# A second buffer for transposed probabilities, an earlier copy, and a layer norm with interleaved subtractions: a transformer sequence block on one Trainium2 core

## The chip, the cores and the metric

The kernel runs on one core of one Trainium2 chip. The metric is device time in microseconds (us), the median of several runs. The five engines are TensorE (PE; its weight loads are shown as PEld), VectorE (DVE), ScalarE (ACT), GpSimd (POOL) and SyncE (SP, which here only issues DMAs). Each engine takes its instructions in the order in which the kernel gives them, and they wait for each other with semaphores.

## The reference

```python
scores = (q @ k.T) / sqrt(D), masked        # 4 batches, 8 heads, 576 tokens, D = 64
attn = exp(scores - rowmax); attn /= attn.sum()
x = heads side by side of (attn @ v)        # [4, 576, 512]
h = gelu(x @ w_in); u, v = halves of h      # 512 each
v_n = (v - mean) / sqrt(var + 1e-6) * g_ln  # layer norm over 512 features
v_s = w_sg @ v_n + b_sg                     # "spatial": mixes the 576 tokens
x = x + (u * v_s) @ w_out
xn = layer norm of x * g2
out = x + relu(xn @ w_ch1) @ w_ch2          # 2048 hidden features
```

Heads 0 to 3 see a local window of 32 tokens, heads 4 to 7 see earlier tokens of the same class (position modulo 32).

## The kernel before

Every product but those of attention is done in three matmuls: each operand is split in a rounded part (hi) and the rest (lo), and hi*hi, hi*lo and lo*hi are summed in PSUM (lines 935 to 937). Making a lo part is one subtraction on DVE or POOL.

Attention of one batch is cut in 24 blocks of 90 to 108 queries for two heads; two blocks make a twin, so a batch has 12 twins, 3 for each pair of heads. A twin s goes through these steps: `scores` (PE, 4 matmuls, line 959), `maxima` (DVE, masked scores to SBUF and row maxima, 722), `exps` (ACT, 4 exponentials and their row sums, 528), `normalise` (DVE, reciprocal 730 and 4 scalings 735), `transposes` (PE, into the one bank `pT_bank`, 972), `copy_pT` (ACT, from that bank to the SBUF tile `probsT`, 538), `values` (PE, into `pv_bank`, 986), `copy_x` (545 on ACT for even twins, 742 on DVE for odd ones) and, once for each pair, `round_x` (DVE, 749) and `split_x` (POOL, 385), which give the operands xop_hi and xop_lo of the next product.

The attention of batch 0 has nothing to run beside it: this is the solo stage, with 15 steps (`SOLO_STEPS`). In step s PE does scores of twin s, transposes of twin s-2 and values of twin s-3, with some warm-up matmuls on zeros (line 943) in steps 0 to 7. A part of the v projection is put between transposes and values in steps 8, 9, 11, 12 and 14 (`SOLO_V`): a v part (k, tokens) is three matmuls, for pair k and one tile of 128 tokens, and needs xop_lo of pair k. The list `REST_V` holds the v parts that SOLO_V does not name; they follow the solo stage. The five v groups (tiles of tokens) are then complete, eight u groups follow, and their Gelu runs on ACT.

Then comes the layer norm of v in five tiles (`norm_all_v` on DVE: `v_stats` lines 753 and 756, `v_norm` lines 760 and 763; on POOL `root_v`, lines 392 and 395, and `split_v`, line 400). In POOL's queue before it stand split_x and the four `split_win` of the u half (line 374); in DVE's queue before it stand four casts (710) and `split_wsg`, the five subtractions that split the spatial weights w_sg (830 and 835). The first mix group (the product with w_sg) waits for all five wsg_lo and for all five vn_lo. On PE the scores of twin 0 of the next batch stand just ahead of it.

From there on, the attention of batch b+1 is interleaved with the mix and out groups of batch b (`period`), by the lists `AFTER_T` and `AFTER_P`: each step holds scores, transposes, one or two groups, and values. DVE finishes a mix group in `gate` (770 and 774), POOL makes gated_lo (407). In the first period POOL also splits w_out (379) right after the layer norm. After four batches comes the feed-forward product in six tiles of 384 tokens, the larger part of the span.

Of the kernel before, what the change touches and what calls it, by code (L numbers as in the profile page):

```python
# [16 lines left out]
F32 = mybir.dt.float32  # L17
F32R = mybir.dt.float32r
BF16 = mybir.dt.bfloat16
ALU = mybir.AluOpType  # L20
# [3 lines left out]
P = 128  # L24
# [29 lines left out]
for _pair in range(PAIRS // 2, PAIRS):  # L54
    for _i, _n in enumerate(CLASSES):
# [5 lines left out]
TWINS = NT // 2  # L61
# [4 lines left out]
NS = -(-S // P)  # L66
LAST = S - (NS - 1) * P
# [18 lines left out]
LAG = 2  # L86
STEPS = TWINS + LAG
# [1 line left out]
SOLO_LAG = LAG + 1  # L89
SOLO_STEPS = TWINS + SOLO_LAG  # L90

SOLO_V = {8: ((0, 0), (0, 1)), 9: ((0, 2), (0, 3)), 11: ((1, 0), (1, 1)), 12: ((1, 2), (1, 3)),
          14: ((2, 0), (2, 1))}

def warm_steps(s):
    return 3 if s < LAG else 2 if s < min(SOLO_V) else 0


REST_V = [(k, s) for k in range(KC) for s in range(NS - 1) if (k, s) not in sum(SOLO_V.values(), ())]
AFTER_T = [(0,), (1,), (2,), (3,), (5,), (6,), (7,), (8,), (10,), (11,), (12,), (13,), (14,), (15,)]  # L100
# [5 lines left out]
def sequence_block_kernel(nc, qT, kT, vW, w_in, g1, w_sgT, b_sg, w_out, g2, w_ff, masks, eye, out):  # L106
    with ExitStack() as ctx:
        def sb(name, shape, dt=F32, stack=ctx):
            return stack.enter_context(nc.sbuf_tensor(name, shape, dt))

        def sem(name):
            return ctx.enter_context(nc.semaphore(name))
# [8 lines left out]
        phase_a = ExitStack()  # L121
# [1 line left out]
        k_sb = sb("k_sb", [P, PAIRS, KPAD], F32, phase_a)  # L123
        v_sb = sb("v_sb", [P, NT, P], F32, phase_a)
        probs = sb("probs", [P, 3, 4 * P], F32, phase_a)
        probsT = sb("probsT", [P, 4 * P], F32, phase_a)
        win_hi = sb("win_hi", [P, KC, 2 * GATE], F32R, phase_a)
        win_lo = sb("win_lo", [P, KC, 2 * GATE], F32R, phase_a)
        xop_hi = sb("xop_hi", [P, KC, S], F32R, phase_a)
# [3 lines left out]
        wsg_hi = sb("wsg_hi", [P, NS, S], F32R, phase_a)  # L133
# [34 lines left out]
        wsg_raw_last = res[:, S:2 * S]  # L168
# [37 lines left out]
        mask_in, class_mask_in, eye_in, const_in = sem("mask_in"), sem("class_mask_in"), sem("eye_in"), sem("const_in")  # L206
# [7 lines left out]
        win_hi_ready, wrest_hi_ready = sem("win_hi_ready"), sem("wrest_hi_ready")  # L214
        wa_lo = sem("wa_lo")
        wsg_lo_ready = sem("wsg_lo_ready")
# [6 lines left out]
        pv_ready = sem("pv_ready")  # L223
# [51 lines left out]
        pT_bank, pv_bank = bank[2], bank[3]  # L275
# [26 lines left out]
        def settle(engine):  # L302
            engine.sem_inc(waited, 1)
# [219 lines left out]
        def _(act):  # L523
            def exps(b, s):
                for j in range(2):
                    act.wait_ge(max_ready, b * NT + (2 * s + j + 1))
                    for h in range(2):
                        last = act.activation(probs_at(s, j, h), probs_at(s, j, h), ACT.Exp, scale=-1.0,  # L528
                                              bias=stat_at(neg_max, s, j, h),
                                              accum_out=stat_at(row_sum, s, j, h))  # L530
                    last.then_inc(exp_done, 1)

            def copy_pT(b, s):
                _, nq, nk, _, _, _ = BLOCKS[2 * s]
                if s >= 1:
                    act.wait_ge(pv_ready, b * TWINS + s)
                act.wait_ge(pT_ready, b * TWINS + (s + 1))
                act.activation(probsT[0:nk, 0:4 * nq], pT_bank[0:nk, 0:4 * nq],
                               ACT.Copy).then_inc(pT_copied, 1)

            def copy_x(b, s):
                dst, src = heads_out(b, s)
                act.wait_ge(pv_ready, b * TWINS + (s + 1))
                settle(act)
                act.activation(dst, src, ACT.Copy).then_inc(x_even, 1)
# [102 lines left out]
                norm_hi(0, 0)  # L648

            for s in range(SOLO_STEPS):  # L650
                if s < TWINS:
                    exps(0, s)
                if LAG <= s < STEPS:
                    copy_pT(0, s - LAG)
                if s >= SOLO_LAG and s % 2 == SOLO_LAG % 2:
                    copy_x(0, s - SOLO_LAG)
            period(0, first=True)
# [37 lines left out]
        def _(dve):  # L695
# [16 lines left out]
            def maxima(b, s):  # L712

                _, nq, nk, _, _, _ = BLOCKS[2 * s]
                dve.wait_ge(scores_ready, b * TWINS + (s + 1))
                if s >= 3:
                    dve.wait_ge(pT_ready, b * TWINS + (s - 2))
                settle(dve)
                for j in range(2):
                    mask = mask_b[0:nq, BLOCKS[2 * s + j][5], 0:nk]  # L720
                    for h in range(2):
                        last = dve.tensor_tensor_reduce(out=probs_at(s, j, h), in0=scores_at(s, j, h),  # L722
                                                        in1=mask, scale=-SCALE, scalar=3.0e38, op0=ALU.add,
                                                        op1=ALU.min, accum_out=stat_at(neg_max, s, j, h))
                    last.then_inc(max_ready, 1)
# [25 lines left out]
            def v_stats(b, s):  # L751
                dve.wait_ge(gelu_done, b * NGELU + (s + 1))
                dve.bn_stats(bn6[:, s, :], gv[:, s, :]).then_inc(bn_done, 1)
                dve.wait_ge(bn_done, b * NS + (s + 1))
                settle(dve)
                dve.bn_aggr(mean_var[:, s, :], bn6[:, s, :]).then_inc(aggr_done, 1)

            def v_norm(b, s):
                dve.wait_ge(rstd_done, b * NS + (s + 1))
                dve.tensor_scalar(gv[:, s, :], gv[:, s, :], mean_var[:, s, 0:1],  # L760
                                  rstd_v[:, s:s + 1], ALU.subtract, ALU.mult).then_inc(vn_done, 1)
                dve.wait_ge(vn_done, b * NS + (s + 1))
                dve.tensor_copy(vn_hi[:, s, :], gv[:, s, :]).then_inc(vnh_ready, 1)
# [20 lines left out]
            def empty_group(b, i):  # L784
                if i < NMIX:
                    gate(b, i)
                else:
                    add_out(b, i - NMIX)
# [28 lines left out]
                    dve.tensor_tensor(w_lo[f][:, part], w_raw[:, f % 2, part], w_hi[f][:, part].bitcast(F32),  # L817
                                      ALU.subtract).then_inc(done, 1)

            def norm_all_v(b):  # L820
                for s in range(NS + 1):
                    if s < NS:
                        v_stats(b, s)
                    if s >= 1:
                        v_norm(b, s - 1)

            def split_wsg():
                for s in range(NS - 1):
                    dve.wait_ge(wrest_hi_ready, s + 1)
                    dve.tensor_tensor(wsg_lo[:, s, :], wsg_raw[:, s, :],  # L830
                                      wsg_hi[:, s, :].bitcast(F32), ALU.subtract).then_inc(wsg_lo_ready, 1)

                dve.wait_ge(wrest_hi_ready, NS)
                second = wsg_hi[LAST:P, NS - 1, :]
                dve.tensor_tensor(second, wsg_raw_last[LAST:P, :], second.bitcast(F32),
                                  ALU.subtract).then_inc(wsg_lo_ready, 1)
                dve.wait_ge(const_in, 48)

            def period(b, first=False):
                if first:  # L840
                    split_wsg()
                norm_all_v(b)
                for s in range(STEPS):
                    if s < TWINS:
                        maxima(b + 1, s)
                    if 1 <= s <= TWINS:
                        normalise(b + 1, s - 1)
                    if s % PER_PAIR == LAG and s > LAG:
                        round_x(b + 1, s // PER_PAIR - 1)
                    for i in AFTER_T[s]:  # L850
                        empty_group(b, i)
                    if s >= LAG and s % 2 != LAG % 2:
                        copy_x(b + 1, s - LAG)
                    for i in AFTER_P[s]:
                        empty_group(b, i)
                round_x(b + 1, PAIRS - 1)
# [73 lines left out]
        def _(pe):  # L930
# [44 lines left out]
            def values(b, s):  # L975
                _, nq, nk, _, _, _ = BLOCKS[2 * s]
                if s % PER_PAIR == 0:
                    pe.wait_ge(v_in[s // PER_PAIR], (b + 1) * 16)
                if s >= 1:
                    wait_copied(pe, b, s - 1)  # L980
                pe.wait_ge(pT_copied, b * TWINS + (s + 1))
                settle(pe)
                for j in range(2):
                    for h in range(2):
                        rows = slice(h * D, (h + 1) * D)
                        last = pe.matmul(pv_bank[rows, j * nq:(j + 1) * nq], v_sb[0:nk, 2 * s + j, rows],  # L986
                                         probsT[0:nk, (2 * j + h) * nq:(2 * j + h + 1) * nq], start=True, stop=True)
                last.then_inc(pv_ready, 1)

            def v_part(b, s, chunks, first=False):  # L990
# [111 lines left out]
            for s in range(SOLO_STEPS):  # L1102
# [7 lines left out]
                warm_up(warm_steps(s) - warm_steps(s) // 2)  # L1110
                for k, tokens in SOLO_V.get(s, ()):
                    v_part(0, tokens, (k,), first=True)
# [122 lines left out]
```

## Time and profile before

| | |
|---|---|
| time, median of 3 runs | 736.11 us (732.35 to 737.01) |
| the profiled execution, time | 732.36 us |
| the profiled execution, span | 730.6 us |
| PE busy | 712.1 us (97%) |
| DVE, ACT, POOL busy | 331.6, 251.5, 195.8 us |
| mean granted clock of TensorE | 0.997 of full |

The span runs from the first to the last instruction that the profile shows; the time has 1.8 us more around it. Times in rows are microseconds from the span's start. Busy PE time is modelled, since matmuls overlap.

### The profile page before, as it was taken

The page shows a single profiled execution, that of the slowest core. Times are in us where ns is not written, and L with a number is a line of the kernel's source. Part 1 is how long each engine was busy: PE and PEld are TensorE (multiplying, and loading weights), DVE is VectorE, ACT ScalarE, POOL GpSimd, SP SyncE. Part 2 cuts the span into 40 slices and gives each one's busy share as a digit, 9 for nine tenths or more (in the row PEclk, how much of TensorE's full clock was granted, in tenths as well). Part 3 has the DMA queues.
Part 4 walks back from the last instruction along what each step waited for, and adds up shares of the span by engine and source line. Part 5 has one row for each costly group of instructions (what it writes and reads, how often), then busy time and mean ns, then how long its engine had stood idle before and what let it go on. Part 6 is the DMA issues. An engine that isn't in the chain of part 4 may idle for free.

```text
span 730.6 us, 12914 instructions
## 1 busy us (share of the span) xinstructions
PE 712.1 (97%) x4768; PEld 669.4 (92%) x4768; DVE 331.6 (45%) x1032; ACT 251.5 (34%) x738; POOL 195.8 (27%) x194
## 2 busy tenths in 40 slices
PE   8778999999999999999999999999999999999998
PEld 4558888988898888999999999999999999999998
DVE  6857883688468846673442231223222222322112
ACT  6754563376337634434431211122112112121110
POOL 1347321622162236463350203020201302010000
PEclk9999999999999999999999999999999999999999
DMA  8541004200420010024301000100100010001001
GB/s 300 205 164 58 1 1 142 80 2 1 132 89 0 0 58 1 31 74 145 126 33 44 1 1 0 44 1 1 44 1 1 0 44 1 1 1 44 1 0 44
DMA packets 15992, 35.02 MB, mean 48 GB/s; under 512 B 1728, under 2 KB 5696, under 8 KB 15936
## 3 DMA queue, kind: packets, MB, share of 16 engines
q1 hardware_dynamic: 15936, 34.29, 13.3%
q8 instruction: 34, 0.56, 0.3%
q14 instruction: 22, 0.18, 0.1%
HBM read 29.56 MB, written 4.72 MB: 47 GB/s over the span
## 4 chain that ended last, share of the span: by engine, by line
PE 91%; DVE 4%; POOL 2%; issue 2%; ACT 1%; DVEq 0%; POOLq 0%; ACTq 0%
PE bank L935 27%; PE bank L937 27%; PE bank L936 27%; PE bank L959 3%; PE bank L986 3%; PE bank L972 3%; DVE probs L722 1%; DVE probs L735 1%; DVE wsg_lo L830 1%; PE bank L943 1%; PE bank L1049 1%; PE bank L1050 1%; POOL rstd_v L395 0%; POOL vn_lo L400 0%; ACT probs L528 0%
## 5 line engine op out<-in xcount | busy, mean ns | idle before, releaser
L898 DVE SCALAR_TENSOR_TENSOR hid_lo<-bank,hid_hi 128x384 fp32r<-128x384 f32 x96 | 53.5, 557 | 281.0 <-ACT hid_hi L664 281.0
L664 ACT ACTIVATE hid_hi<-bank 128x384 fp32r<-128x384 f32 x96 | 47.1, 491 | 300.7 <-PE bank L937 300.7
L936 PE MATMUL bank<-xn_lo,w_hi 128*128 128x384 f32 x384 | 129.5, 337 | 0.0
L937 PE MATMUL bank<-hid_hi,w_lo 128*128 128x384 f32 x384 | 129.5, 337 | 0.0
L935 PE MATMUL bank<-hid_hi,w_hi 128*128 128x384 f32 x384 | 129.4, 337 | 0.0
L937 PE MATMUL bank<-xn_hi,w_lo 128*128 128x384 f32 x384 | 129.2, 336 | 0.0
L935 PE MATMUL bank<-xn_hi,w_hi 128*128 128x384 f32 x384 | 129.0, 336 | 0.0
L936 PE MATMUL bank<-hid_lo,w_hi 128*128 128x384 f32 x384 | 128.9, 336 | 0.0
L528 ACT ACTIVATE probs<-probs,stat 96x128 f32<-96x128 f32 (+2 forms) x192 | 71.9, 377 | 9.6 <-DVE stat L722 9.4
L935 PEld LDWEIGHTS bank<-hid_hi,w_hi 128*128 128x128 f32 x384 | 72.2, 188 | 0.0
L937 PEld LDWEIGHTS bank<-xn_hi,w_lo 128*128 128x128 f32 x384 | 72.1, 188 | 0.0
L935 PEld LDWEIGHTS bank<-xn_hi,w_hi 128*128 128x128 f32 x384 | 72.1, 188 | 0.0
L936 PEld LDWEIGHTS bank<-hid_lo,w_hi 128*128 128x128 f32 x384 | 72.1, 188 | 0.0
L936 PEld LDWEIGHTS bank<-xn_lo,w_hi 128*128 128x128 f32 x384 | 72.1, 188 | 0.0
L937 PEld LDWEIGHTS bank<-hid_hi,w_lo 128*128 128x128 f32 x384 | 72.0, 188 | 0.0
L722 DVE CUSTOM_DVE_ANT_0 probs<-bank,mask_b 96x128 f32<-96x128 f32 (+2 forms) x192 | 41.1, 266 | 20.0 <-PE bank L959 18.9
L440 POOL TENSOR_TENSOR xn_lo<-xc,xn_hi 128x1536 fp32r<-128x1536 f32 x6 | 21.1, 3511 | 100.2 <-ACT xn_hi L597 100.2
L735 DVE TENSOR_SCALAR probs<-probs,stat 96x128 f32<-96x128 f32 (+2 forms) x192 | 46.1, 299 | 1.8
L407 POOL TENSOR_TENSOR gated_lo<-u_sb,gated_hi 128x288 fp32r<-128x288 f32 x32 | 27.2, 854 | 62.7 <-ACT gated_hi L574 62.7
L385 POOL TENSOR_TENSOR xop_lo<-res,xop_hi 128x576 fp32r<-128x576 f32 x16 | 22.7, 1416 | 78.1 <-DVE xop_hi L749 78.1
L935 PE MATMUL bank<-wsg_hi,vn_hi 128*128 128x288 f32 x128 | 40.3, 315 | 3.1 <-POOL vn_lo L400 3.1
L935 PE MATMUL bank<-gated_hi,wout_hi 128*128 128x288 f32 x128 | 39.9, 311 | 0.0
(97 smaller groups left out, 1338.7 us busy)
## 6 DMA issues: line engine op xcount, KB each, us to landing
w_raw<-w_ff_dram SPq DMA_DIRECT2D x16, 512.0 KB, 3.5
v_sb<-vW_dram SPq DMA_DIRECT2D x16, 384.0 KB, 6.7
k_sb<-kT_dram SPq DMA_DIRECT2D x15, 304.0 KB, 6.8
q_sb<-qT_dram SPq DMA_DIRECT2D x15, 288.0 KB, 6.5
out_dram<-res SPq DMA_DIRECT2D x5, 768.0 KB, 3.9
res<-w_sgT_dram SPq DMA_DIRECT2D x1, 1152.0 KB, 10.7
win_v_raw<-w_in_dram SPq DMA_DIRECT2D x4, 256.0 KB, 6.8
win_u_raw<-w_in_dram SPq DMA_DIRECT2D x4, 256.0 KB, 8.7
```

The source lines that it names most:

```text
L385: pool.tensor_tensor(xop_lo[:, pair, :], res_at(b, pair, 0, S), xop_hi[:, pair, :].bitcast(F32), ALU.subtract).then_inc(x_lo, 1)
L407: pool.tensor_tensor(gated_lo[:, c, cols], u_sb[:, c, cols], gated_hi[:, c, cols].bitcast(F32), ALU.subtract).then_inc(gl_ready, 1)
L528: last = act.activation(probs_at(s, j, h), probs_at(s, j, h), ACT.Exp, scale=-1.0, bias=stat_at(neg_max, s, j, h), accum_out=stat_at(row_s ...
L664: act.activation(hid_hi[:, f % 2, :], h_bank[f % 2][:, 0:TILE], ACT.Relu).then_inc(hh_ready, 1)
L722: last = dve.tensor_tensor_reduce(out=probs_at(s, j, h), in0=scores_at(s, j, h), in1=mask, scale=-SCALE, scalar=3.0e38, op0=ALU.add, op1=A ...
L735: last = dve.tensor_scalar(e, e, stat_at(row_inv, s, j, h), None, ALU.mult)
L898: dve.scalar_tensor_tensor(out=hid_lo[:, f % 2, :], in0=h_bank[f % 2][:, 0:TILE], scalar=0.0, in1=hid_hi[:, f % 2, :].bitcast(F32), op0=AL ...
L935: pe.matmul(dst, wh, xh, start=(start and i == 0), stop=False)
L936: pe.matmul(dst, wh, xl, start=False, stop=False)
L937: last = pe.matmul(dst, wl, xh, start=False, stop=(stop and i == n - 1))
L959: last = pe.matmul(scores_at(s, j, h), q_sb[rows, pair, q0:q0 + nq], k_sb[rows, pair, k0:k0 + nk], start=True, stop=True)
L972: last = pe.transpose(pT_bank[0:nk, cols], probs_at(s, j, h), eye_f[0:nq, 0:nq])
```

## The change

- `probsT` gets two buffers; twin s uses number s % 2. `copy_pT` of twin s then waits for the values of twin s-2 instead of s-1, in all periods.
- In the solo stage ACT does `copy_pT` of twin s-2 ahead of `exps` of twin s; it stood behind them. In the other periods the copy stood ahead already.
- The five subtractions for w_sg no longer precede the layer norm of v in DVE's queue. One follows each of its iterations. The wait for the constants moves behind the layer norm.
- The two v parts of step 14 of the solo stage go to `REST_V`, behind it.

```diff
-SOLO_V = {8: ((0, 0), (0, 1)), 9: ((0, 2), (0, 3)), 11: ((1, 0), (1, 1)), 12: ((1, 2), (1, 3)),
-          14: ((2, 0), (2, 1))}
+SOLO_V = {8: ((0, 0), (0, 1)), 9: ((0, 2), (0, 3)), 11: ((1, 0), (1, 1)), 12: ((1, 2), (1, 3))}
...
-        probsT = sb("probsT", [P, 4 * P], F32, phase_a)
+        probsT = sb("probsT", [P, 2, 4 * P], F32, phase_a)
...
             def copy_pT(b, s):
-                if s >= 1:
-                    act.wait_ge(pv_ready, b * TWINS + s)
+                if s >= 2:
+                    act.wait_ge(pv_ready, b * TWINS + (s - 1))
                 act.wait_ge(pT_ready, b * TWINS + (s + 1))
-                act.activation(probsT[0:nk, 0:4 * nq], pT_bank[0:nk, 0:4 * nq],
+                act.activation(probsT[0:nk, s % 2, 0:4 * nq], pT_bank[0:nk, 0:4 * nq],
...
             for s in range(SOLO_STEPS):
+                if LAG <= s < STEPS:
+                    copy_pT(0, s - LAG)
                 if s < TWINS:
                     exps(0, s)
-                if LAG <= s < STEPS:
-                    copy_pT(0, s - LAG)
...
-            def norm_all_v(b):
+            def norm_all_v(b, first=False):
                 for s in range(NS + 1):
                     if s < NS:
                         v_stats(b, s)
                     if s >= 1:
                         v_norm(b, s - 1)
+                    if first and s < NS:
+                        split_wsg(s)
...
             def period(b, first=False):
+                norm_all_v(b, first)
                 if first:
-                    split_wsg()
-                norm_all_v(b)
+                    dve.wait_ge(const_in, 48)
```

## Rows read from the trace of the kernel before

**Rows 1.** Waits of PE over the whole span: total us, times, longest us.

```profile
PE bank L972 <- ACT probsT L538: 5.1, 9, 1.0
...
PE bank L935 <- POOL xop_lo L385: 2.7, 2, 1.4
```

**Rows 2.** Windows: length, busy PE, PEld, DVE, ACT, POOL, PEclk, DMA share, GB/s.

```profile
71.30:74.50 3.20, 3.20 (x19) 2.64 (x17) 0.96 (x2) 0.00 (x0) 3.20 (x4) 0.50 0.02 5
...
200.00:260.00 60.00, 60.00 (x515) 53.38 (x513) 45.03 (x199) 35.30 (x132) 20.35 (x25) 1.00 0.09 33
```

**Rows 3.** Timeline of ACT, solo stage: start, us, instruction, idle before and its releaser.

```profile
11.40 0.47 ACT L538 ACTIVATE probsT<-bank 128x384 f32<-128x384 f32 x1
...
39.67 0.47 ACT L538 ACTIVATE probsT<-bank 90x360 f32<-90x360 f32 x1 [2.25 <-PE bank L986]
```

**Rows 4.** Timeline of PE, solo stage to the first mix groups.

```profile
12.01 0.52 PE L972 MATMUL bank<-eye_f,probs 96*128 96x96 f32 x4 [0.63 <-ACT probsT L538]
...
25.26 0.55 PE L972 MATMUL bank<-eye_f,probs 108*108 108x108 f32 x4 [1.54 <-DVE probs L735]
...
34.05 0.55 PE L972 MATMUL bank<-eye_f,probs 108*108 108x108 f32 x4 [1.01 <-ACT probsT L538]
...
37.19 0.48 PE L972 MATMUL bank<-eye_f,probs 90*90 90x90 f32 x4 [0.72 <-ACT probsT L538]
...
39.03 0.59 PE L986 MATMUL bank<-probsT,v_sb 108*64 108x108 f32 x8
...
42.68 0.47 PE L935 MATMUL bank<-win_hi,xop_hi 128*128 128x512 f32 x1 [1.34 <-POOL xop_lo L385]
...
44.24 0.53 PE L986 MATMUL bank<-probsT,v_sb 90*64 90x90 f32 x8
...
47.75 0.47 PE L935 MATMUL bank<-win_hi,xop_hi 128*128 128x512 f32 x1 [1.39 <-POOL xop_lo L385]
...
53.72 0.40 PE L935 MATMUL bank<-xop_hi,win_hi 128*128 128x288 f32 x1 [0.23 <-POOL win_lo L374]
...
70.45 0.37 PE L935 MATMUL bank<-wsg_hi,vn_hi 128*128 128x288 f32 x1 [3.13 <-POOL vn_lo L400]
```

**Rows 5.** Timeline of DVE, solo stage: the scalings of twins 1 and 9.

```profile
10.36 0.87 DVE L735 TENSOR_SCALAR probs<-probs,stat 96x128 f32<-96x128 f32 x4
...
32.46 0.83 DVE L735 TENSOR_SCALAR probs<-probs,stat 108x108 f32<-108x108 f32 x4
```

**Rows 6.** Timeline of DVE: three w_sg subtractions (narrow windows), then the layer norm's start.

```profile
50.67 1.85 DVE L830 TENSOR_TENSOR wsg_lo<-res,wsg_hi 128x576 fp32r<-128x576 f32 x1
...
54.20 1.42 DVE L830 TENSOR_TENSOR wsg_lo<-res,wsg_hi 128x576 fp32r<-128x576 f32 x2
...
56.44 0.69 DVE L753 BATCH_NORM_STATS2 bn<-gv 128x6 f32<-128x512 f32 x1
...
57.38 0.66 DVE L753 BATCH_NORM_STATS2 bn<-gv 128x6 f32<-128x512 f32 x1
...
58.58 0.55 DVE L760 TENSOR_SCALAR gv<-gv,mean_var,rstd_v 128x512 f32<-128x512 f32 x1 [0.20 <-POOL rstd_v L395]
59.16 0.43 DVE L763 CAST vn_hi<-gv 128x512 fp32r<-128x512 f32 x1
```

**Rows 7.** Timeline of POOL: u half of w_in, then vn_lo of tiles 1, 2 and 4.

```profile
47.57 6.10 POOL L374 TENSOR_TENSOR win_lo<-win_u_raw,win_hi 128x512 fp32r<-128x512 f32 x4
...
62.09 1.29 POOL L400 TENSOR_TENSOR vn_lo<-gv,vn_hi 128x512 fp32r<-128x512 f32 x1
...
64.53 1.28 POOL L400 TENSOR_TENSOR vn_lo<-gv,vn_hi 128x512 fp32r<-128x512 f32 x1
...
69.04 1.26 POOL L400 TENSOR_TENSOR vn_lo<-gv,vn_hi 128x512 fp32r<-128x512 f32 x1 [0.82 <-DVE vn_hi L763]
```

**Rows 8.** Timeline of DVE and PE: the first gate's product, the first period's first transposes.

```profile
74.05 1.51 DVE L774 TENSOR_TENSOR u_sb<-gt,u_sb 128x288 f32<-128x288 f32 x1
...
77.73 0.52 PE L972 MATMUL bank<-eye_f,probs 96*128 96x96 f32 x4 [0.42 <-DVE probs L735]
```

More of the change, by code:

```diff
@@ L825, in norm_all_v, with split_wsg @@
                         v_norm(b, s - 1)
-            def split_wsg():
-                for s in range(NS - 1):
-                    dve.wait_ge(wrest_hi_ready, s + 1)
+                    if first and s < NS:
+                        split_wsg(s)
+            def split_wsg(s):
+                dve.wait_ge(wrest_hi_ready, s + 1)
+                if s < NS - 1:
                     dve.tensor_tensor(wsg_lo[:, s, :], wsg_raw[:, s, :],
                                       wsg_hi[:, s, :].bitcast(F32), ALU.subtract).then_inc(wsg_lo_ready, 1)
[L833 to L837, printed above, removed]
+                else:
+                    second = wsg_hi[LAST:P, NS - 1, :]
+                    dve.tensor_tensor(second, wsg_raw_last[LAST:P, :], second.bitcast(F32),
+                                      ALU.subtract).then_inc(wsg_lo_ready, 1)
             def period(b, first=False):
+                norm_all_v(b, first)
                 if first:
-                    split_wsg()
-                norm_all_v(b)
+                    dve.wait_ge(const_in, 48)
                 for s in range(STEPS):
@@ L986, in values @@
                         last = pe.matmul(pv_bank[rows, j * nq:(j + 1) * nq], v_sb[0:nk, 2 * s + j, rows],
-                                         probsT[0:nk, (2 * j + h) * nq:(2 * j + h + 1) * nq], start=True, stop=True)
+                                         probsT[0:nk, s % 2, (2 * j + h) * nq:(2 * j + h + 1) * nq], start=True, stop=True)
                 last.then_inc(pv_ready, 1)
```

## The prediction

> **What bounds the kernel now.** I read the waits of PE first. PE is busy 712.1 of 730.6 us, so the change can only give back idle time, and nearly all of that is early: 5.1 us in nine waits of transposes for the copy of the transposed probabilities and 2.7 us in two waits of v parts for xop_lo [rows 1], and 3.13 us in one wait of the first mix group for vn_lo [rows 4]. The windows say where the reader should look: after 80 us PE shows no idle time until the last tail, one short wait aside (60.00 busy in the window of 60.00 between 200 and 260 us) [rows 2]. So every microsecond by which PE reaches the steady part earlier should come off the end, and the changed wait of `copy_pT` in the later periods is worth nothing, since there no PE instruction waits for it. The windows show one more loss: right after the wait of 3.13 us [rows 4] the granted clock is 0.50 (1.2 GHz) from 71.30 to 74.50 [rows 2]. Shorter PE waits, up to 1.54 us [rows 4], are followed by no such fall. At half clock those 3.20 us hold work of 1.6.
>
> The timelines then show the chains. In the solo stage the copy of twin 0 starts at 11.40, behind the exponentials of twin 2, and transposes 1 start at 12.01 after it [rows 3, 4], though their own data left DVE at 10.36 + 0.87 = 11.23 [rows 5]. At the end of the stage there are no exponentials any more, but each copy waits for the values before it (copy 10 after 2.25 us of idle time ended by line 986) [rows 3], each transposes for the copy, and each values for its place behind v parts: a ring of three engines.
>
> **The change part by part.** I walk along PE and note by how much each landmark of [rows 4] comes sooner (its shift).
>
> 1. Copy ahead of exponentials. Transposes 1 can start 0.11 after the scalings, at 11.34 instead of 12.01: shift 0.7. What is late next is DVE's own order (maxima, scalings), which sets the pace up to transposes 6: these wait 1.54 us for the scalings, not for a copy [rows 4], so the shift there is still 0.7 and the other early copy waits give nothing. The exponentials are now queued behind the copy (0.38 of ACT's time each step) and behind the transposes it waits for. I cost that at nothing, as the scalings of a twin come a whole step later on DVE, and at 0.4 for twins 2 and 8 at worst.
>
> 2. Two buffers. Transposes 7 and 8 lose short waits, 0.35 together (part of the nine): shift 1.05. Transposes 9 at 34.05 waited 1.01 for copy 8. Without that they wait for scalings 9, which end at 32.46 + 0.83 = 33.29 [rows 5], plus 0.11, less the 1.0 by which the twin is early: 32.4, shift 1.6. From 9 to 10 there is then only PE work: 3.14 apart less the 0.72 of waiting [rows 4] gives 2.42, so transposes 10 start at 34.8 and values 9 (1.84 behind them as before) at 36.6: shift 2.4. Transposes 11 follow at 37.1, copy 11 at 37.7 while values 10 run, values 11 at 38.3 instead of 44.24: shift 5.9. The 5.9 includes the 1.5 us of two v parts that no longer stand ahead of it.
>
> 3. The two v parts. They need xop_lo of pair 2, which hangs on values 9 through copy_x 9, round_x and split_x. They now start at 42.68 - 2.4 = 40.3. Four parts of pair 2 (0.70 each, from two in about 1.4) take PE to 43.1. xop_lo of pair 3 hangs on values 11 and comes at 47.75 - 5.9 = 41.8, under them. So the wait of 1.39 goes and pair 3's parts start at 43.1: shift 4.65. A wait of about 1.5 us stays between values 11 and 40.3. The u groups lose a further 0.23 of waiting for win_lo, if that is ready: it ended at 47.57 + 6.10 = 53.67 [rows 7], hangs on values 11 too, and so comes at 47.8, ahead of the u groups at 48.85 (shift 4.9). PE was ready for the first mix group at 70.45 - 3.13 = 67.32 [rows 4] and would be at 62.45.
>
> 4. Subtractions in the layer norm. Before, DVE did them from 50.67 to 56.4 and only then the statistics [rows 6]. Now statistics 0 start when Gelu of the first v group is done, near 44.8, and the gate is POOL: its win_lo ends at 47.8, rstd of tile 0 is there a microsecond later, near 48.8 (the same two POOL operations fill the 1.15 between the end of vn_lo 1 at 63.38 and vn_lo 2 [rows 7]). From there the chain is scalings and cast of tile 0 (1.1), a subtraction of 0.7 (two in 1.42 where nothing collides) [rows 6], vn_lo 0 to 51.65, then three turns, then 2.1 for the last tile: vn_lo 3 to vn_lo 4, as now. A turn took 64.53 - 62.09 = 2.44 [rows 7], set by POOL, with DVE waiting inside it. DVE's work in a turn (0.94 from one statistics to the next, 0.55 scalings, 0.43 cast, 0.71 subtraction [rows 6]) is 2.6, so I take 2.65. Three turns give 59.6, the last tile 61.7, the mix group 61.85: 0.6 ahead of PE. Bounds: 2.44 a turn if it hides fully (61.2), and 0.94 + 0.55 + 0.43 + 1.85 = 3.8 if each subtraction, tile 0's too, takes the 1.85 of the colliding one at 50.67 [rows 6] (a mix group at 51.65 + 1.15 + 3 x 3.8 + 2.1 + 0.15 = 66.4). I stay near the low end, because that row collided with POOL subtractions back to back, 6.10 us for four, and in the layer norm POOL runs one of 1.29 per turn [rows 7].
>
> The rows show what a collision is: two subtractions, one on DVE and one on POOL, never progress together; 1.85 is 1.2 of waiting and 0.7 of work. The Trainium skill ("SBUF — State Buffer", "Who interferes with whom") says the same as a rule: a DVE instruction with two SBUF inputs and a GpSimd instruction that reads SBUF take an exclusive lock, and the second one is fully blocked. It speaks against this edit, since it moves DVE's subtractions from beside win_lo to beside vn_lo. By that rule a turn is at least the locked work of both, which gives an estimate of about 2.9 to 3.0 and a mix group at 62.8, 0.4 late on PE; without any lock, 2.6 and no wait.
>
> 5. First period. With the mix group at 62.45 (shift 8.0) the 3.13 wait is gone and so, by the only case there is, the fall of the clock: 1.6 more. It isn't all kept. At full clock DVE is late: the first gate's product took 1.51 [rows 8], beside POOL's splits of w_out, which still follow vn_lo. Mix group 0 ends at 64.4, gate to 66.45, maxima 1 to 67.4, scalings 0 to 68.4, transposes 0 at 68.55 instead of 77.73 [rows 8]: shift 9.2. If the gate's product doesn't collide, 67.7 and a shift of 10.
>
> From transposes 0 on the steps are those of before. The sum: 2.4 (attention until values 9), 2.25 (v parts), 0.25 (win_lo), 3.1 (layer norm), 1.2 (clock, less DVE's lateness) = 9.2. I take 9.1. The profiled execution, 732.36 with a span of 730.6, would become 723.3. It is near the lowest of the runs; the median is 3.75 above it. I take the saving off the median: 736.1 - 9.1 = **727.0**.
>
> **The rivals.** (a) The layer norm stays last. With turns of 3.8 the mix group starts at 66.4, PE waits 4.0 us, the clock falls again, and the gain ends where it stands at that group: 4.0, time 732.1. For it: the 1.85 row and the one wide vector instruction more in every turn. Against: POOL is free of subtractions for half a turn. A turn of 3.1 costs only 0.7 and stays in my range.
>
> (b) The solo stage is held by DVE and ACT, not by copies. Before, transposes 6 wait for DVE [rows 4]; if scalings 9 to 11 come late too (exponentials behind copies, scalings that collide with POOL), values 11 gain 3 instead of 5.9, win_lo and the layer norm follow, and the gain is 5 to 6: time 730.5.
>
> (c) Slower. The clock falls ahead of the u groups. The two v parts no longer fill the wait for xop_lo at the end of the solo stage, and PE idles there. I get 1.5 us; the clock fell after 3.13 and not after 1.54 [rows 4], so it decides if round_x or split_x of pair 2 come 1.5 us later relative to values 11. If the clock then stayed at half for all of the v parts and u groups, 40.3 to 62.4, that would be 22 us more, and 749. For it: PE has idle time all through this stage. Against: the one fall of the trace lasted 3.2 us and cost 1.6, and that much would leave 728.6. Only a long fall makes it slower.
>
> (d) The second buffer doesn't act: there is still one `pT_bank`, so transposes s+1 wait for copy s anyway. That wait is now only the copy's 0.47 after the transposes, under other PE work except at twins 10 and 11, so I give the buffer its effect. If it fell out, parts 1, 3 and 4 remain, some 5 us: 731.
>
> **How the numbers follow.** Forecast, gain 7.4 to 10.5: 0.66. (a) 0.11. (b) and (d) together, 4 to 7.3: 0.17. (c) 0.03. No visible effect because something unseen takes its place: 0.03. The range reaches from the highest gain on the lowest level of the runs (732.4 - 10.5 = 722) to (a) and (b) on the median's level, 732. A measurement of this kernel tells about 1% (7.4 us) from no change. Faster by over 1%: 0.65; within 1%: 0.32, from (a), (b), (d) and the low end of the forecast; slower: 0.03.
>
> **What would show it.** Right: no PE wait for line 538 in twins 9 to 11 of the solo stage; values 11 near 38.3; one wait for xop_lo left, of about 1.5 us; the wait for vn_lo under 1 us; granted clock 1.00 around the first mix group; transposes 0 of the first period near 68.6; every later landmark earlier by the same amount. Wrong: subtractions of 1.8 us each inside the layer norm, with vn_lo turns over 3.5; a wait of transposes for line 735 that grows in twins 9 to 11; a half clock anywhere between 38 and 62 us.

## The result and the profile after

The changed kernel takes 724.43 us (median of 4 runs, 724.2 to 725.51) against 734.23 (4 runs, 732.28 to 737.01) for the kernel before. The ratio is 0.9867, with a 95% interval of 0.9825 to 0.9909. In a later set of runs on one chip it was 726.28 against 734.78, ratio 0.9886 (0.9862 to 0.9910). The profiled executions have spans of 722.4 and 730.6 us: 8.2 less, where the prediction said 9.1 to 9.2.

The waits of PE in the changed kernel, over the whole span (lines have moved up by one: 971 are transposes, 985 values, 958 scores, 934 to 936 the three products):

```profile
PE bank L971 <- issue: 2.8, 4, 1.6
PE bank L958 <- DVE stat L721: 1.9, 5, 0.5
...
PE bank L985 <- ACT res L544: 1.0, 2, 0.7
PE bank L985 <- DVE res L741: 0.7, 1, 0.7
PE bank L971 <- DVE probs L734: 0.5, 1, 0.5
```

Of the three kinds of wait of [rows 1] and [rows 4] none is left: no transposes wait for the copy, no v part for xop_lo, and the mix group doesn't wait for vn_lo. The transposes that wait with no releaser shown ("issue") are those of twins 1, 4, 6 and 9, the 1.6 being that of twin 6, which waited for DVE's scalings before [rows 4]. One kind has grown: scores wait for DVE's maxima, 1.9 us in five waits where it was 0.8 in two; this is the other ring of the solo stage. One is new: values wait for `copy_x`, lines 544 and 741. The prediction had one wait for xop_lo of about 1.5 us left. There is none, because values 11, 1.5 us later than it said, stand in that time.

The timelines of DVE (first line, the scalings of twin 9) and PE show where each landmark of [rows 4] went:

```profile
31.57 0.83 DVE L734 TENSOR_SCALAR probs<-probs,stat 108x108 f32<-108x108 f32 x4
...
32.50 0.55 PE L971 MATMUL bank<-eye_f,probs 108*108 108x108 f32 x4 [0.35 <-issue]
...
36.72 0.59 PE L985 MATMUL bank<-probsT,v_sb 108*64 108x108 f32 x8
...
38.49 0.53 PE L985 MATMUL bank<-probsT,v_sb 90*64 90x90 f32 x8 [0.74 <-DVE res L741]
39.77 0.53 PE L985 MATMUL bank<-probsT,v_sb 90*64 90x90 f32 x8 [0.75 <-ACT res L544]
40.37 0.50 PE L934 MATMUL bank<-win_hi,xop_hi 128*128 128x512 f32 x1
...
44.78 0.39 PE L934 MATMUL bank<-win_hi,xop_hi 128*128 128x512 f32 x1
...
50.28 0.29 PE L934 MATMUL bank<-xop_hi,win_hi 128*128 128x288 f32 x1
...
63.70 0.40 PE L934 MATMUL bank<-wsg_hi,vn_hi 128*128 128x288 f32 x1
...
69.56 0.52 PE L971 MATMUL bank<-eye_f,probs 96*128 96x96 f32 x4 [0.46 <-DVE probs L734]
```

| landmark | before | walked in the prediction | after |
|---|---|---|---|
| transposes 9 | 34.05 | 32.4 | 32.50 |
| values 9 | 39.03 | 36.6 | 36.72 |
| values 11 | 44.24 | 38.3 | 39.77 |
| first v part of pair 2 behind the stage | 42.68 | 40.3 | 40.37 |
| first v part of pair 3 | 47.75 | 43.1 | 44.78 |
| u groups | 53.72 | 48.85 | 50.28 |
| first mix group | 70.45 | 62.45 | 63.70 |
| transposes 0, first period | 77.73 | 68.55 | 69.56 |

The last row is 8.17 us earlier and the end 8.2: behind it nothing was gained or lost, as PE has no idle time there.

The clock did not stay at full. The window of the changed kernel that answers to that of [rows 2] (same columns) is

```profile
40.60:44.00 3.40, 3.40 (x9) 2.69 (x9) 3.27 (x5) 3.07 (x5) 2.29 (x2) 0.51 0.69 224
```

PE's clock was 0.51 of full here (the third number from the end). The fall behind the layer norm is gone and another stands here, after a stretch (37.2 to 40.4) of short PE work with waits of 0.74 and 0.75. A half clock anywhere between 38 and 62 us was one of the prediction's own signs of being wrong.

The layer norm of v with its subtractions, DVE (two turns) and POOL:

```profile
51.14 0.75 DVE L831 TENSOR_TENSOR wsg_lo<-res,wsg_hi 128x576 fp32r<-128x576 f32 x1
...
53.71 0.75 DVE L831 TENSOR_TENSOR wsg_lo<-res,wsg_hi 128x576 fp32r<-128x576 f32 x1
...
56.27 0.75 DVE L831 TENSOR_TENSOR wsg_lo<-res,wsg_hi 128x576 fp32r<-128x576 f32 x1
```

```profile
43.10 6.13 POOL L373 TENSOR_TENSOR win_lo<-win_u_raw,win_hi 128x512 fp32r<-128x512 f32 x4
...
51.30 1.74 POOL L399 TENSOR_TENSOR vn_lo<-gv,vn_hi 128x512 fp32r<-128x512 f32 x1
...
54.19 1.42 POOL L399 TENSOR_TENSOR vn_lo<-gv,vn_hi 128x512 fp32r<-128x512 f32 x1
...
61.70 1.29 POOL L399 TENSOR_TENSOR vn_lo<-gv,vn_hi 128x512 fp32r<-128x512 f32 x1 [0.83 <-DVE vn_hi L762]
```

A subtraction takes 0.75, not 1.85; vn_lo pays for it, 1.74 and 1.42 instead of 1.29. A turn is 2.57 (51.14 to 53.71, and again to 56.27). The last vn_lo ends at 61.70 + 1.29 = 62.99, 0.7 us ahead of the first mix group at 63.70.

Behind the mix group, DVE's first gate product and the scalings of twin 0:

```profile
66.41 0.62 DVE L773 TENSOR_TENSOR u_sb<-gt,u_sb 128x288 f32<-128x288 f32 x1
...
68.00 1.42 DVE L734 TENSOR_SCALAR probs<-probs,stat 96x128 f32<-96x128 f32 x4
```

### The profile page after: what moved, and what is told of

Read it like the earlier page. It is cut to its first block, busy times and chain, and to the rows that moved or that the text cites. A ratio compares the mean times of both kernels' runs of the same rounds, so it can differ in the third digit from the quotient of the medians.

```text
span 722.4 us, 12909 instructions
## 1 busy us (share of the span) xinstructions
PE 710.7 (98%) x4766; PEld 669.7 (93%) x4768; DVE 327.9 (45%) x1032; ACT 251.4 (35%) x738; POOL 197.0 (27%) x194
## 4 chain that ended last, share of the span: by engine, by line
PE 95%; DVE 3%; issue 1%; POOL 1%; ACT 0%; DVEq 0%; POOLq 0%; ACTq 0%
PE bank L934 28%; PE bank L935 28%; PE bank L936 28%; PE bank L958 3%; PE bank L985 3%; PE bank L971 3%; DVE probs L721 1%; DVE probs L734 1%; PE bank L1048 1%; PE bank L942 1%; PE bank L1049 1%; PE bank L1054 0%; DVE res L905 0%; PE bank L1055 0%; POOL acc L419 0%
```

## The experiments

Times vary by up to 3 or 4 us between executions of one kernel, and the first thing to learn from the runs was why. "Half clock" below is a granted clock of 0.50, which is 1.2 GHz. Each execution comes with its mean granted clock. Spans of the executions for which that clock is on record, by clock:

| kernel | 1.000 | 0.998, 0.997 | 0.995 | 0.993 | 0.991 |
|---|---|---|---|---|---|
| before | | 730.5 to 731.3 | 731.4 to 733.1 | 732.2 to 734.4 | 734.4 to 734.6 |
| changed | | 722.4 to 722.7 | 723.7 to 725.4 | | |
| v parts kept | | 725.7 to 726.1 | 727.7 | | |
| exponentials first | 723.7 | | 725.4 | 726.4, 726.9 | |
| one buffer | | | 727.2, 727.3 | 728.0, 728.1 | |
| w_sg first | | 725.2 | 725.8, 726.5 | 727.6 | |
| attention only | | 728.8 | 729.0 to 729.6 | 730.5 | |
| spread only | 726.7 | 727.7, 728.1 | 729.6 to 730.1 | | |
| v parts only | | | 729.4, 729.7 | 730.0 to 731.2 | 731.1 |
| other pv bank | 721.3 | 722.2 | 723.6 | 724.9 | |
| warm-up in the tail | 722.3, 722.7 | 723.5, 724.0 | | | |
| bank and warm-up | 721.3 to 721.6 | | 724.2, 724.3 | | |
| more warm-up | 721.4 to 721.6 | | | | |

The windows of the profiled executions show what a column means: 1.000 has no half clock, 0.998 one stretch of some 3.4 us, 0.995 twice as much in all (in two stretches, or in one of 6.8 us), 0.993 three times. Within a row, each 3.4 us at half clock go with 0.8 to 1.7 us more. So I compare within a column. That still leaves up to 2 us open, as in the row of the changed kernel at 0.995 (723.7 twice, 725.3 twice and 725.4): where the stretches lie counts too. The differences below are of that precision.

**1. Undoing one part at a time.** The v parts:

```diff
+          14: ((2, 0), (2, 1))}
```

> The changed kernel with the two v parts of pair 2 back in step 14, ahead of values 11. Theory (the v parts held values 11, and with them pair 3's operand and POOL's win_lo): values 11 move from 39.8 to about 41.8, xop_lo of pair 3 ends near 45.2 and is waited for again, the u groups start near 51.4 instead of 50.3, the first mix group waits a little for vn_lo, span about 723.9 (1.5 more than the changed kernel's 722.4). Rival (values 11 are held by the one pv bank anyway, so the order is free): span 722.4.

Measured: ratio to before 0.9920 (0.9893 to 0.9947), span 725.7, 3.3 more than the changed kernel at the same clock: twice what the theory said.

```profile
43.10 0.62 PE L986 MATMUL bank<-probsT,v_sb 90*64 90x90 f32 x8
46.70 0.47 PE L935 MATMUL bank<-win_hi,xop_hi 128*128 128x512 f32 x1 [1.40 <-POOL xop_lo L385]
...
66.47 0.37 PE L935 MATMUL bank<-wsg_hi,vn_hi 128*128 128x288 f32 x1 [0.21 <-POOL vn_lo L400]
```

Values 11 come at 43.10 instead of 39.77, 3.3 later, since the two parts ahead of them wait for xop_lo until 40.27 and then run at half clock. xop_lo of pair 3, POOL's four win_lo, rstd and vn_lo hang on values 11 in one row, and the last vn_lo is 3.3 later too. The mix group moved by 2.77 only, from 63.70 to 66.47, since PE had reached it 0.7 us behind vn_lo. The rest was lost behind it, at the first gate's product, which meets POOL's splits of w_out in both kernels.

```profile
72.90 0.52 PE L972 MATMUL bank<-eye_f,probs 96*128 96x96 f32 x4 [0.85 <-DVE probs L735]
```

The product (line 774, at 69.17) took 1.21 for 0.62 and transposes 0 waited 0.85 for 0.46, so they ran at 72.90 for 69.56: 3.3 again, as the end. That it is the same 3.3 as at values 11 is thus in part chance.

The order on ACT:

```diff
-                if LAG <= s < STEPS:
-                    copy_pT(0, s - LAG)
                 if s < TWINS:
                     exps(0, s)
+                if LAG <= s < STEPS:
+                    copy_pT(0, s - LAG)
```

> The changed kernel with the exponentials ahead of the copy again in the solo stage, two buffers kept. Theory (the order is what transposes 1 and 9 gained by): transposes 1 at 12.0 again, transposes 9 near 34.0 instead of 32.5, all later landmarks 1.5 later, span 723.9. Rival (DVE sets the pace of the solo stage and the order gives nothing that lasts): transposes 9 near 32.7, span 722.6.

Measured: 0.9903 (0.9872 to 0.9934). The profiled execution had a wait of 1.2 for k_sb's DMA and three falls of the clock, so its landmarks are late for other reasons. Its waits are plain:

```profile
PE bank L971 <- ACT probsT L537: 2.7, 4, 1.0
```

The longest of the four is that of transposes 9, 1.01 as before the change, although there are two buffers. What this costs is less sure. The run without a fall has a span of 723.7. The changed kernel has no such run; the kernel with warm-up in the tail (below), the nearest to it, has 722.3 and 722.7, and those that also use the other bank 721.3 to 721.6. At 0.995 it has 725.4 against 723.7 to 725.4. The order is thus worth some 1 to 2 us; the theory's 1.5 fits, and the rival, by which the order gives nothing that lasts, does not fit the waits that came back.

One buffer:

```diff
-                if s >= 2:
-                    act.wait_ge(pv_ready, b * TWINS + (s - 1))
+                if s >= 1:
+                    act.wait_ge(pv_ready, b * TWINS + s)
```

(and index 0 in place of s % 2)

> The changed kernel with one buffer for the transposed probabilities: copy s waits for values s-1 again. Theory (values 10 and 11 now wait for the copy of the values before them out of the one pv bank, so a second buffer can give little): transposes 10 about 0.7 later, values 11 near 40.4 instead of 39.8, span 723.1. Rival (the buffer is what broke the ring, as the prediction had it): values 11 near 42, span 725 or more.

Measured: 0.9937 (0.9912 to 0.9961), 727.2 and 727.3 at clock 0.995, where the changed kernel has 723.7 to 725.4: 2 to 3.5 more. My theory of 0.7 fell. PE and ACT in the solo stage:

```profile
33.48 0.61 PE L985 MATMUL bank<-probsT,v_sb 90*64 90x90 f32 x8 [1.40 <-ACT res L544]
...
44.27 0.87 PE L985 MATMUL bank<-probsT,v_sb 90*64 90x90 f32 x8 [1.02 <-ACT res L544]
```

```profile
30.98 0.47 ACT L537 ACTIVATE probsT<-bank 90x360 f32<-90x360 f32 x1 [1.21 <-PE bank L985]
31.35 0.37 ACT L527 ACTIVATE probs<-probs,stat 108x108 f32<-108x108 f32 x1
...
32.82 0.52 ACT L544 ACTIVATE res<-bank 128x216 f32<-128x216 f32 x1
```

Copy 7 waits 1.21 for values 6, and the exponentials of twin 9, ready earlier, stand behind it in ACT's queue; behind those stands `copy_x` 6, for which values 7 wait 1.40. With the copy moved ahead of the exponentials, its wait holds all that stands behind it on ACT. Values 11 came at 44.27, later than even the rival's 42, with two stretches at half clock on the way. So I take it that the early copy needs the second buffer. The changed kernel with both edits undone would test it; it was not run.

The subtractions in one piece:

```diff
                 if first:
+                    for s in range(NS):
+                        split_wsg(s)
-                    if first and s < NS:
-                        split_wsg(s)
```

> The changed kernel with the five subtractions for w_sg in one piece ahead of the layer norm again. Theory (they delay the first statistics by 5.7, and the layer norm sets when the first mix group starts): statistics 0 near 52, first mix group near 66.0 instead of 63.7 after a PE wait of 2.3, span 724.7, and 726 if the clock falls there too. Rival (spreading only moves the same work, as DVE is busy either way): span 722.4 to 723.

Measured: 0.9921 (0.9895 to 0.9947), span 725.2 at clock 0.998: 2.8 more.

```profile
65.94 0.37 PE L935 MATMUL bank<-wsg_hi,vn_hi 128*128 128x288 f32 x1 [2.29 <-POOL vn_lo L399]
```

Statistics 0 at 51.9, mix group at 65.94, wait 2.29: the theory's 52, 66.0 and 2.3. The clock did not fall behind this wait of 2.29.

**2. One part alone, on the kernel before.**

Attention only, which is two buffers and the copy ahead of the exponentials:

```diff
-                if s >= 1:
-                    act.wait_ge(pv_ready, b * TWINS + s)
+                if s >= 2:
+                    act.wait_ge(pv_ready, b * TWINS + (s - 1))
...
+                if LAG <= s < STEPS:
+                    copy_pT(0, s - LAG)
                 if s < TWINS:
                     exps(0, s)
-                if LAG <= s < STEPS:
-                    copy_pT(0, s - LAG)
```

> The kernel before with the second buffer and the earlier copy alone: v parts in step 14, w_sg subtractions ahead of the layer norm. Theory (parts of the gain add up along one chain): values 9 near 36.7 as in the changed kernel, first mix group near 68 after a PE wait of about 3, span 728.5 against 730.6 before. Rival (the attention part alone gives nothing, as the layer norm then takes it back): span 730 or more.

The spread subtractions only:

```diff
+                    if first and s < NS:
+                        split_wsg(s)
```

> The kernel before with the spread w_sg subtractions alone (one buffer, exponentials first, v parts in step 14). Theory: rstd of tile 0 comes 0.95 after win_lo's end at 53.7, so vn_lo 4 ends near 67.5 and the first mix group starts near 67.6 instead of 70.45, with no fall of the clock; transposes 0 of the first period gain 3.5, span 727.1. Rival (the turns of the layer norm lengthen by the whole collision, to 3.8): first mix group near 71, span 731.

The v parts only:

```diff
-          14: ((2, 0), (2, 1))}
```

> The kernel before with the two v parts of pair 2 moved behind the solo stage, and nothing else. Theory (what counts is when values 11 run, since xop_lo of pair 3, win_lo and the layer norm hang on them): copy 11 stays at 41.4, values 11 near 41.9 instead of 44.24, everything behind win_lo 2.3 sooner, span 728.2 at one fall of the clock, 2.3 less than before. Rival (the v parts filled an idle stretch, so moving them costs their own 1.4): span 732.

Measured ratios: 0.9958 (0.9941 to 0.9975), 0.9942 (0.9921 to 0.9962), 0.9974 (0.9959 to 0.9990). In the column of 0.998 attention alone has 728.8 and the spread alone 727.7 to 728.1, against 730.5 to 731.3: about 2 (1.7 to 2.5) and 3 us (2.4 to 3.6). The v parts alone have 729.4 and 729.7 at 0.995, against 731.4 to 733.1, about 2.5 (1.7 to 3.7). The theories' spans (728.5, 727.1, 728.2) were written for executions with one or no fall of the clock, and hold there for the first (728.8) and second (726.7 without a fall). None of the ten runs of the third came to 728.2. The profiled executions had three stretches, two, and one of 6.8 us. In the spread-only kernel the first mix group starts 0.9 behind the scores at 69.94, with a wait of 0.21: the 3.13 of [rows 4] are gone by this edit alone. In the kernel with the moved v parts alone values 11 ran at 42.56 (theory 41.9, plus a wait for `copy_x`) and the mix group still waited 3.15.

The parts alone add up to about 7.5 us (5.8 to 9.8), together they give 7.8 to 8.9 in the column of 0.998. They add up within that precision; whether they help each other can't be read from it.

**3. The tail of the solo stage.** The values of twin 10 into a bank that is free then:

```diff
+        def pv_of(b, s):
+            return bank[1] if isinstance(b, int) and b == 0 and s == TWINS - 2 else pv_bank
...
+                if pv_of(b, s) is not pv_bank:
+                    pe.wait_ge(max_ready, NT)
+                elif s >= 2 and pv_of(b, s - 1) is not pv_bank:
+                    wait_copied(pe, b, s - 2)
-                if s >= 1:
+                elif s >= 1:
                     wait_copied(pe, b, s - 1)
```

> The changed kernel with the values of twin 10 in another PSUM bank in the solo stage, so that values 10 and 11 do not wait for copies out of the one pv bank. Theory (that bank is the wait the prediction overlooked): both waits of 0.74 go, values 11 near 38.3, xop_lo of pair 3 1.4 earlier. The pair 2 parts stay near 40.4, since they hang on values 9, so the span changes by what the clock does: 722.4 if it falls again, 720.8 if it does not. Rival (values 11 wait for something else): values 11 stay near 39.8.

Measured: 0.9881 (0.9851 to 0.9910), span 722.2.

```profile
37.68 0.53 PE L993 MATMUL bank<-probsT,v_sb 90*64 90x90 f32 x8
38.49 0.53 PE L993 MATMUL bank<-probsT,v_sb 90*64 90x90 f32 x8 [0.28 <-DVE res L745]
40.37 0.57 PE L938 MATMUL bank<-win_hi,xop_hi 128*128 128x512 f32 x1 [1.34 <-POOL xop_lo L388]
```

Values 11 at 38.49, as walked in the prediction (38.3), and the wait of 1.34 for xop_lo that it foresaw. The clock falls again at 40.6 and the span is the same: the bank was what held values 11, and on its own it isn't worth anything, since PE reached the mix group behind vn_lo already and still does (63.71).

Warm-up matmuls in the waits (three ahead of values 10 and of values 11; in the second kernel, with the other bank, six behind values 11 instead):

```diff
+                if s >= TWINS + 1:
+                    pe.wait_ge(max_ready, NT)
+                    warm_up(3, bank[0])
                 if SOLO_LAG <= s:
                     values(0, s - SOLO_LAG)
...
+            warm_up(6, bank[0])
```

> The changed kernel with three warm-up matmuls (zeros, into a free bank) ahead of values 10 and three ahead of values 11. Theory (PE's idle stretches between 37 and 40.4 make the clock fall at 40.6, which costs 1.6): no half clock, u groups at 48.7, but vn_lo hangs on values 11 through win_lo and ends at 63.0 as now, so the first mix group only comes 0.6 sooner: span 721.8. Rival (the clock falls whatever PE does there): 722.4 or, if the matmuls stand in the way, 723.

> Both: values of twin 10 in another bank, and six warm-up matmuls after values 11, in the wait for xop_lo of pair 2. Theory: no half clock (1.6 less) and vn_lo 1.4 earlier, so the first mix group starts near 62.1 instead of 63.7, span 720.8 and a time near 722.6. Rival (the rest is bound elsewhere, by the first gates on DVE): span 722.

Measured: 0.9875 (0.9852 to 0.9898) and 0.9865 (0.9841 to 0.9889). In the profiled execution of neither is there a half clock between 37 and 50. The first reaches 722.3 and 722.7 in its runs without any fall, no better than the changed kernel with one: vn_lo still hangs on values 11 (the mix group waits 0.23 for it), and behind it transposes 0 wait 0.85 for DVE where it was 0.46. The second reaches 721.3 to 721.6. That is the theory's order, though the first was put at 721.8 and the second at 720.8; the wait of 0.85 is there too, so the rival, the gates on DVE, took a part. But in the profiled executions of both the clock now fell earlier, from 24.4 to 27.8 us in the first (724.0) and from 24.0 to 30.8 in the second (724.3).

The same fall was then found in the changed kernel itself, run again:

> The changed kernel once more. Theory (the spread between executions is the number of times the clock falls, each about 1.0 to 1.6 us): span 722.4 at a mean granted clock of 0.998, 723.7 at 0.995, and never 1.000, as the fall at 40.6 is always there. Rival (the spread is something else): span and mean clock unrelated.

```profile
24.78 0.94 PE L971 MATMUL bank<-eye_f,probs 108*108 108x108 f32 x4 [1.65 <-issue]
...
25.20:31.50 6.30, 6.30 (x32) 4.72 (x31) 3.17 (x22) 2.44 (x11) 1.17 (x1) 0.55 0.49 172
```

This execution, of 725.3, has the half clock from 24.05, inside the wait, to 30.85, and none at 40.6 (mean 0.995). In the profiled one of 722.4 the same wait of 1.65 stands at 24.57 and nothing follows it. The theory holds in part: there is one fall or more in all ten executions of the changed kernel, but not always the same one, and at 0.995 two spans are the 723.7 it gave and three are 725.3 or 725.4.

So the last kernel also fills that wait:

```diff
+                if s == min(SOLO_V):
+                    warm_up(5, bank[7])
                 if LAG <= s < STEPS:
                     transposes(0, s - LAG)
```

> The changed kernel with the other bank for the values of twin 10, six warm-up matmuls behind values 11, and five more ahead of transposes 6, where PE waits 1.65 for DVE. Theory: no fall between 24 and 32 either, mean clock 1.000 in all executions, span 721.4, time 723.1, about 1.3 less than the changed kernel. Rival (falls come elsewhere then): mean clock 0.998 or less in half of the executions, 722 to 724.

Two of its windows, then the first mix group and transposes 0 of the first period:

```profile
20.00:32.00 12.00, 10.75 (x105) 7.24 (x107) 10.44 (x60) 8.47 (x39) 5.36 (x4) 1.00 0.71 257
32.00:64.00 32.00, 31.29 (x223) 26.23 (x220) 24.21 (x64) 19.07 (x45) 22.82 (x23) 1.00 0.36 127
```

```profile
62.29 0.37 PE L938 MATMUL bank<-wsg_hi,vn_hi 128*128 128x288 f32 x1
...
68.72 0.52 PE L975 MATMUL bank<-eye_f,probs 96*128 96x96 f32 x4 [0.86 <-DVE probs L738]
```

723.27 us, ratio to before 0.9850 (0.9827 to 0.9873), granted clock 1.000 in all five runs, and times between 723.16 and 723.34: the spread of 1.3 to 3 us is gone, and the median is 3.0 under that of the changed kernel in the same set (726.28), 1.2 under its median in the first set. It is the fastest version of this study. Without any fall the mix group comes 1.4 sooner than in the changed kernel, at 62.29, and transposes 0 only 0.84 sooner: a part of what the full clock gives back is lost again in the longer wait for DVE, 0.86 for 0.46.

## Why the prediction was right, and where not

**Direction, size, cause.** The idle time of the first 78 us was what could be given back, and everything won there came off the end. The gain of 9.2 was 8.2 in the profiled span. Term by term, from the landmarks:

| term | predicted | measured |
|---|---|---|
| attention until values 9 | 2.4 | 2.31 |
| v parts and win_lo, until the u groups | 2.5 | 1.13 |
| layer norm, until the first mix group | 3.1 | 3.31 |
| first period, until its transposes 0 | 1.2 | 1.42 |
| sum | 9.2 | 8.17 |

So the term that was mis-sized is that of the v parts, by 1.4. The median fell from 736.1 to 724.4, by more than the 9.1, but 736.1 came from three executions of before. With a fourth it is 734.23, and over the later sets 733.7 to 734.9. The number 727.0 erred mostly there: off 734.23 the same saving gives 725.1.

**Copy and buffer (2.4 at values 9).** Right, 36.72 for 36.6, with the reason given: transposes 9 came to be held by DVE's scalings, which end at 31.57 + 0.83 = 32.40, and start at 32.50. Undoing the two halves singly cost some 1 to 2 and 2 to 3.5. I had not seen how much the halves need each other. The step "the exponentials are now queued behind the copy" was rightly costed at nothing, as the changed kernel has the second buffer; with one buffer it is not so.

**Values 11 (38.3).** Wrong by 1.5. The step "copy 11 at 37.7 while values 10 run, values 11 at 38.3" looked at transposes and copy and overlooked the other single bank: values s wait for `copy_x` s-1, written in `values` as `wait_copied`. Before, those waits were hidden under the waits for the copy. The run with the other bank puts it right to 0.2.

**The two v parts (2.25).** The mechanism was right, what they cover and that the wait for pair 3 goes. Pair 3's parts came at 44.78 instead of 43.1, and this is the clock's 1.6, not the order: the stretch from 40.6 to 44.0 lies on them. What values 11 are worth depends on who comes last at the mix group. Later by 3.3, they moved the mix group by 2.8 and the end by 3.3; earlier by 1.3 (the other bank), they moved the end by 0.2, as PE was then the last.

**Layer norm (3.1).** Right: turns of 2.57 for 2.65, mix group without a wait. Rival (a) with 3.8 fell, as the 0.75 per subtraction shows, and so did the estimate of 2.9 to 3.0, by which a turn is at least the locked work of both engines. The subtraction at 53.71 ran beside POOL's `root_v` for 0.5 of its 0.75 us, and neither took longer than elsewhere. The operation that pays is POOL's vn_lo, 0.13 in two turns, 0.26 and 0.45 in the others with a subtraction. The 0.6 us by which vn_lo was to come ahead of PE held, but by luck: vn_lo 4 ended at 62.99 for 61.7, with values 11 behind it, and PE was held back by the half clock. With warm-up in the tail, where that half clock is gone and values 11 come as long after values 9, the mix group does wait for vn_lo, 0.23 us. In the prediction's start of this chain the terms written (48.8, 1.1, 0.7 and a vn_lo of 1.29) add up to 51.9, not 51.65; the trace has 2.86 from rstd to the end of vn_lo 0, as the 51.65 has.

**The clock (1.2).** Here a step failed. "Shorter PE waits, up to 1.54 us, are followed by no such fall" was read from a single execution. In other executions it falls in a wait of 1.65, and after two of 0.75 with little work between. So the fall behind the layer norm did go, and the term for it came out (1.42 for 1.2), but one at 40.6 or at 24 came in its place, and the 1.6 was given back in the term of the v parts. Rival (c) had the place of it (the v parts behind the solo stage) and the size of the short form, 1.6; the long form that would have made the kernel slower was not seen, the longest stretch being 6.8 us.

**The first period (transposes 0 at 6.1 behind the first mix group).** They came 5.9 behind it. DVE's lateness cost PE 0.46 there, as foreseen in kind; the first gate's product took 0.62 instead of 1.51, but the scalings behind it took 1.42 for four, 1.06 before the change.

What stays open: why the clock falls in the same wait of 1.65 in one execution and not in the next. The runs show only that there was no fall in five executions of five once both stretches were filled with matmuls on zeros.

## What to carry to other kernels

When a buffer is doubled to break a ring of engines, list every single-buffered step of the ring first: the next one becomes the wait, and it is invisible as long as the first one covers it. An operation moved ahead in a queue brings its waits with it, so the move and the buffer that shortens its wait are best made as one edit. Work put ahead of the last link of a serial chain through other engines (here values 11, then xop_lo, win_lo, vn_lo) costs its delay at the end wherever that chain is what comes last, however idle PE is meanwhile; where another engine comes last, shortening the chain gives nothing (722.2 for 722.4).

## What was not expected of the hardware

Most of the spread between executions of one kernel, 730.5 to 734.6 us for the kernel before, goes with the time at half clock: by the mean clock one to four times 3.4 us, at different places from run to run, each worth 0.8 to 1.7. It can come in one piece: 24.05 to 30.85 us in one execution of the changed kernel. The clock fell within a wait of 1.65 us in one execution and not in the other, and not at a wait of 2.29. At a wait of 3.15 (v parts only) it stayed at half for 6.8 us, at one of 3.13 in the kernel before for 3.4. Eleven warm-up matmuls in two PE waits, with the other bank, made five executions agree within 0.2 us.

POOL and DVE subtractions that meet do not both slow down: DVE kept 0.75 and POOL's 1.29 became 1.42 to 1.74. By the Trainium skill ("SBUF — State Buffer", "Who interferes with whom") the port pair that the two share is an exclusive lock, and the order of issue decides who blocks. The trace agrees: only the later one is longer, and of the subtractions in the layer norm the later one is POOL's. At 51.30 it started 0.59 us before DVE's ended (51.14 + 0.75) and took 0.45 longer; at 54.19 it was 0.27 and 0.13. So it loses the overlap, less 0.14. Where DVE was the later one it paid:

```profile
59.75 1.42 DVE L759 TENSOR_SCALAR gv<-gv,mean_var,rstd_v 128x512 f32<-128x512 f32 x1
...
59.32 1.55 POOL L399 TENSOR_TENSOR vn_lo<-gv,vn_hi 128x512 fp32r<-128x512 f32 x1
```

The same scaling takes 0.55 to 0.59 in the other turns.
